# Token-mixer kernel: rows of the middle stage on every fourth partition, its tables in eight parts, stores ahead of loads

## Time and profile before

| | before |
|---|---|
| median of three runs | 3273.02 us |
| the profiled execution's own time | 3274.27 us |
| its span, first to last instruction | 3272.1 us |
| mean granted TensorE clock | 0.962 |
| TensorE busy | 2991.4 us (91%) |
| VectorE, GpSimd, ScalarE busy | 2595.4, 1578.9, 1297.7 us |
| first matmul of the middle stage | 384.57 us |
| first and last issue of a large store (L442) | 394.66 and 487.82 us |

### The profile page before, as it was taken

How to read it: one execution, slowest core, us unless ns; L and a number is a source line. 1 busy time by engine, 2 the same in 40 slices (tenths; PEclk the granted TensorE clock), 3 DMA queues, 4 the chain that set the end, 5 groups by cost and what they waited for, 6 DMA issues and landing times.

```text
span 3272.1 us, 58005 instructions
## 1 busy us (share of the span) xinstructions
PE 2991.4 (91%) x17218; PEld 2833.4 (87%) x17218; DVE 2595.4 (79%) x4304; ACT 1297.7 (40%) x2452; POOL 1578.9 (48%) x1527
## 2 busy tenths in 40 slices
PE   2555689999999799999999999999999999999999
PEld 2444438989898799999999999999999999999999
DVE  7999566777777888887878788787878788887776
ACT  1111235666667433333333333333333333333443
POOL 5666304666667544544545354444544454443221
PEclk7777799999999899999999999999999999999999
DMA  7656582332333466565656566565656565655443
GB/s 237 205 192 206 154 243 85 110 122 97 113 107 131 164 221 217 214 232 209 224 199 232 209 224 220 203 233 199 236 197 237 211 222 217 222 216 181 142 132 80
DMA packets 212157, 613.21 MB, mean 187 GB/s; under 512 B 19921, under 2 KB 61137, under 8 KB 210833
## 3 DMA queue, kind: packets, MB, share of 16 engines
q1 hardware_dynamic: 202304, 598.04, 52.6%
q10 hardware_dynamic: 9696, 13.37, 1.5%
HBM read 394.67 MB, written 216.66 MB: 187 GB/s over the span
## 4 chain that ended last, share of the span: by engine, by line
PE 75%; issue 8%; POOLq 6%; DVE 4%; DVEq 2%; DMA 2%; ACT 2%; POOL 1%; ACTq 0%; SPq 0%
PE banks L1570 55%; PE banks L1437 10%; POOLq L1042 5%; PE banks L1508 4%; PE banks L1510 2%; DVE zl L797 2%; PE banks L1494 2%; DMA m_scr<-mst 1%; DVEq L845 1%; POOL head L1040 1%; ACT zh L1261 1%; PE banks L1649 1%; DVE angle L785 0%; PE banks L1484 0%; DVE mst L749 0%
## 5 line engine op out<-in xcount | busy, mean ns | idle before, releaser
L1570 PE MATMUL banks<-zh,wh 128*128 128x384 f32 x3828 | 1295.1, 338 | 45.1 <-DVE rbuf L849 45.1
L1570 PE MATMUL banks<-zh,wl 128*128 128x384 f32 x3828 | 1282.1, 335 | 0.0
L1570 PE MATMUL banks<-zl,wh 128*128 128x384 f32 x3828 | 1281.3, 335 | 0.0
L849 DVE TENSOR_TENSOR rbuf<-rbuf,banks 128x384 f32<-128x384 f32 x1168 | 643.1, 551 | 253.5 <-PE banks L1570 216.4
L1570 PEld LDWEIGHTS banks<-zh,wh 128*128 128x128 f32 x3828 | 720.2, 188 | 67.2 <-DVE rbuf L849 47.5
L1570 PEld LDWEIGHTS banks<-zl,wh 128*128 128x128 f32 x3828 | 720.7, 188 | 0.0
L1570 PEld LDWEIGHTS banks<-zh,wl 128*128 128x128 f32 x3828 | 720.0, 188 | 0.0
L1074 POOL TENSOR_TENSOR wsum<-wraw 128x384 f32<-128x384 f32 x176 | 179.6, 1020 | 1107.6 <-DVE wl L792 982.2
L1253 ACT ACTIVATE wh<-wsum 128x384 fp32r<-128x384 f32 x704 | 370.2, 526 | 771.5 <-PE banks L1570 730.0
L792 DVE TENSOR_TENSOR wl<-wsum,wh 128x384 fp32r<-128x384 f32 x664 | 505.3, 761 | 39.1 <-ACT wh L1253 14.3
L1253 ACT ACTIVATE wh<-wraw 128x384 fp32r<-128x384 f32 x528 | 278.0, 527 | 498.5 <-PE banks L1570 498.5
(11 more groups left out here) (141 smaller groups left out, 4260.4 us busy)
## 6 DMA issues: line engine op xcount, KB each, us to landing
wraw<-w_pairs SPq DMA_DIRECT2D x176, 768.0 KB, 6.7
rbuf<-y_scr SPq DMA_DIRECT2D x176, 768.0 KB, 5.7
y_scr<-rbuf SPq DMA_DIRECT2D x160, 768.0 KB, 4.0
xin<-x_pad SPq DMA_DIRECT2D x22, 1728.0 KB, 9.5
z_scr<-zsc SPq DMA_DIRECT2D x33, 768.0 KB, 4.0
zraw<-z_scr SPq DMA_DIRECT2D x33, 768.0 KB, 7.4
x_scr<-x1s SPq DMA_DIRECT2D x22, 576.0 KB, 5.8
t_scr<-tst ACTq DMA_DIRECT2D x44, 288.0 KB, 4.1
```

Of the source, the lines that this page charges most:

```text
L849: dve.tensor_tensor(part, part, dst(k, i), ALU.add).then_inc(r_done, 1)
L1570: last = pe.matmul(dst, l[w][:, q, :], r[par][:, operand, q, :], start=starts and q == 0 and t == 0, stop=q == 2 and t == 2, skip_group_ch ...
```

## The change

- Rows: real row n (below 32) sits on partition 4 n, imaginary row n on 4 n + 1, and the two rows n = 32 on 2 and 3, in `traw`, in the tables (both sides) and in `mst`. `traw`, `mst` and the matmuls' operands and results are 128 partitions wide.
- Tables: `fall` is 128 partitions x 64 x 256 (8 MB) where it was 96 x 64 x 132 (3.1 MB). It is no longer loaded ahead of the first stage's loop: SP's loop is written out and loads an eighth (1 MB) at the end of each of its rounds 2 to 9.
- Memory: `mst1` takes the place of the raw weights `w1_raw`, `w2_raw` and `wt_raw`; ScalarE waits for `cwl_ready` before the middle stage.
- Stores: the large store becomes two DMAs of 384 KB, one for each of the real and imaginary results.
- Order: `load_t(g + 4)` is issued behind `store_b(g)`, and its own wait on `g_ready` is gone.
- VectorE's clearing (L740) covers all 128 partitions of `traw`.

```diff
+    place = np.array([4 * n + w if n < NT - 1 else 2 + w for w in range(2) for n in range(NT)])
+    f_rows = np.zeros((P, P // 2, 2, P))
...
-        traw = [alloc(T, f"traw{s}", [NRZ, 4, B, D]) for s in range(4)]
+        traw = [alloc(T, f"traw{s}", [P, 4, B, D]) for s in range(4)]
...
-        fall = alloc(C, "fall", [NRZ, P // 2, 2 * NR])
-        mst = [alloc(C, f"mst{s}", [NR, 4, B, D]) for s in range(2)]
-        w1_raw = alloc(C, "w1_raw", [P, 2, F])
+        fall = alloc(C, "fall", [P, P // 2, 2 * P])
+        mst = [alloc(C, "mst0", [P, 4, B, D])]
+        R = ExitStack()
+        w1_raw = alloc(R, "w1_raw", [P, 2, F])
+        w2_raw = alloc(R, "w2_raw", [P, HB, D])
+        wt_raw = alloc(R, "wt_raw", [P, 2, D])
+        R.close()
+
+        mst += [alloc(C, "mst1", [P, 4, B, D])]
...
             def load_t(g):
                 s = g % 4
                 for w in range(2):
-                    sp.dma_start(traw[s][64 * w:64 * w + 32].rearrange("p i b d -> p i (b d)"),
+                    sp.dma_start(traw[s][w:P:4].rearrange("p i b d -> p i (b d)"),
                                  t_scr[w, 0:NT - 1, 4 * g:4 * g + 4, :]).then_inc(b_in[s], 16)
-                sp.dma_start(traw[s][32:34].rearrange("p i b d -> p i (b d)"),
+                sp.dma_start(traw[s][2:4].rearrange("p i b d -> p i (b d)"),
...
+                tiles = m_scr[2 * g:2 * g + 2].rearrange("t (i w a) x -> w a (t i) x", i=2, w=2)
...
-                sp.dma_start(m_scr[2 * g:2 * g + 2].rearrange("t (i q) x -> q (t i) x", i=2), rows[0:64]).then_inc(out_b, 16)
-                sp.dma_start(m_scr[NT - 1:NT, 4 * g:4 * g + 4, :], rows[64:65]).then_inc(out_b, 16)
+                for w in range(2):
+                    sp.dma_start(tiles[w], rows[w:P:4]).then_inc(out_b, 16)
+                sp.dma_start(m_scr[NT - 1:NT, 4 * g:4 * g + 4, :], rows[2:3]).then_inc(out_b, 16)
...
-            sp.dma_start(fall[:], f_low).then_inc(f_in, 16)
...
-            with sp.Fori(1, NG) as g:
+            for g in range(1, NG):
                 for h in range(2):
                     load_a(g, h)
                     store_x1(g - 1, h)
+
+                if 1 < g < 10:
+                    part = slice(8 * (g - 2), 8 * (g - 1))
+                    sp.dma_start(fall[:, part], f_low[:, part]).then_inc(f_in, 16)
...
             for g in range(NGB):
-                if g + 4 < NGB:
-                    sp.wait_ge(g_ready, 4 * g + 4)
-                    load_t(g + 4)
...
                 store_b(g)
+                if g + 4 < NGB:
+                    load_t(g + 4)
...
-                dve.memset(traw[s][32:64], 0.0).then_inc(b_zero, 1)
+                dve.memset(traw[s][:], 0.0).then_inc(b_zero, 1)
...
+            act.wait_ge(cwl_ready, 5)
             step_b(0)
...
-            pe.wait_ge(f_in, 16)
+            pe.wait_ge(f_in, 128)
...
-                    pe.matmul(bank[2 * i][0:NR, 0:4 * (L + 2)], fall[:, q, 0:NR], traw[g % 4][:, i, :, 0:L + 2],
+                    pe.matmul(bank[2 * i][:, 0:4 * (L + 2)], fall[:, q, 0:P], traw[g % 4][:, i, :, 0:L + 2],
                               start=True, stop=True)
-                    pe.matmul(bank[2 * i + 1][0:NR, 0:4 * L], fall[:, q, NR:2 * NR], traw[g % 4][:, i, :, L:D],
+                    pe.matmul(bank[2 * i + 1][:, 0:4 * L], fall[:, q, P:2 * P], traw[g % 4][:, i, :, L:D],
```

More of the change, by code:

```diff
@@ L48 @@
 NPAIR = NT // 2
-NRZ = 96
-NR = 2 * NT
 NGB = P // 8
@@ L96, in fourier_constants @@
             f_low[1, :, i, 1, 1] = -np.sin(p2)
[L98 to L102, removed]
+    place = np.array([4 * n + w if n < NT - 1 else 2 + w for w in range(2) for n in range(NT)])
+    f_rows = np.zeros((P, P // 2, 2, P))
+    f_rows[place[:, None, None, None], np.arange(P // 2)[None, :, None, None], np.arange(2)[None, None, :, None],
+           place[None, None, None, :]] = f_low.reshape(2 * NT, P // 2, 2, 2 * NT)
     none = np.zeros((D2, D))
@@ L106, in fourier_constants @@
     return (f_seq.astype(np.float32), f_chan.astype(np.float32), f_rest.astype(np.float32),
-            f_rows.reshape(NRZ, P // 2, 4 * NT).astype(np.float32))
+            f_rows.reshape(P, P // 2, 2 * P).astype(np.float32))
 def row_order():
@@ L227, in token_fourier_mixer @@
         newton = alloc(C, "newton", [P, B])
-        fall = alloc(C, "fall", [NRZ, P // 2, 2 * NR])
-        mst = [alloc(C, f"mst{s}", [NR, 4, B, D]) for s in range(2)]
-        w1_raw = alloc(C, "w1_raw", [P, 2, F])
+        fall = alloc(C, "fall", [P, P // 2, 2 * P])
[6 more added lines that the diff above has]
+        mst += [alloc(C, "mst1", [P, 4, B, D])]
         w1t = alloc(C, "w1t", [P, F], F32R)
         wtt = alloc(C, "wtt", [P, D], F32R)
-        w2_raw = alloc(C, "w2_raw", [P, HB, D])
-        wt_raw = alloc(C, "wt_raw", [P, 2, D])
         C.close()
@@ L311, in stored @@
         def stored(k, groups):
-            return 48 * groups + (0 if k else 16)
+            return 64 * groups + (0 if k else 16)
         up_bank = (2, 3, 4, 5, 2, 3)
@@ L439, in store_b @@
                 rows = mst[g % 2][:].rearrange("p i b d -> p i (b d)")
+                tiles = m_scr[2 * g:2 * g + 2].rearrange("t (i w a) x -> w a (t i) x", i=2, w=2)
                 out_b = m_out[g % 2]
                 sp.wait_ge(m_ready, 4 * g + 4)
-                sp.dma_start(m_scr[2 * g:2 * g + 2].rearrange("t (i q) x -> q (t i) x", i=2), rows[0:64]).then_inc(out_b, 16)
-                sp.dma_start(m_scr[NT - 1:NT, 4 * g:4 * g + 4, :], rows[64:65]).then_inc(out_b, 16)
+                for w in range(2):
+                    sp.dma_start(tiles[w], rows[w:P:4]).then_inc(out_b, 16)
+                sp.dma_start(m_scr[NT - 1:NT, 4 * g:4 * g + 4, :], rows[2:3]).then_inc(out_b, 16)
                 if g == 0:
-                    sp.dma_start(m_scr[NT - 1:NT, P // 2:P // 2 + 1, :], rows[65:66, 0:1]).then_inc(out_b, 16)
-                    sp.dma_start(m_scr[NT - 1:NT, P - 3:P, :], rows[65:66, 3:0:-1]).then_inc(out_b, 16)
-                else:
-                    sp.dma_start(m_scr[NT - 1:NT, P - 3 - 4 * g:P + 1 - 4 * g, :], rows[65:66, ::-1]).then_inc(out_b, 16)
-            sp.dma_start(fall[:], f_low).then_inc(f_in, 16)
+                    sp.dma_start(m_scr[NT - 1:NT, P // 2:P // 2 + 1, :], rows[3:4, 0:1]).then_inc(out_b, 16)
+                    sp.dma_start(m_scr[NT - 1:NT, P - 3:P, :], rows[3:4, 3:0:-1]).then_inc(out_b, 16)
+                else:
+                    sp.dma_start(m_scr[NT - 1:NT, P - 3 - 4 * g:P + 1 - 4 * g, :], rows[3:4, ::-1]).then_inc(out_b, 16)
             sp.dma_start(w1_raw[:, 0, :], w1[0:P, :]).then_inc(cw_in, 16)
@@ L746, in group_b @@
                     even = mst[s % 2][:, i, :, 1:L]
-                    hpart = bank[2 * i + 1][0:NR, 0:4 * L].rearrange("p (b l) -> p b l", b=B)[:, :, 1:L]
+                    hpart = bank[2 * i + 1][:, 0:4 * L].rearrange("p (b l) -> p b l", b=B)[:, :, 1:L]
                     dve.tensor_tensor(mst[s % 2][:, i, :, D - 1:L:-1], even, hpart, ALU.subtract)
@@ L1200, in group_b @@
                     act.activation(mst[s % 2][:, i, :, 0:L + 1],
-                                   bank[2 * i][0:NR, 0:4 * (L + 2)].rearrange("p (b l) -> p b l", b=B)[:, :, 0:L + 1],
+                                   bank[2 * i][:, 0:4 * (L + 2)].rearrange("p (b l) -> p b l", b=B)[:, :, 0:L + 1],
                                    ACT.Copy).then_inc(g_evac, 1)
```

## The result

The changed kernel takes 3247.5 us (median of 4 runs, 3247.42 to 3249.16) against 3273.03 for the kernel before. The ratio is 0.9923, with a 95% interval of 0.9906 to 0.994. The profiled execution has a span of 3245.6 us, 26.5 less than before, and a mean granted TensorE clock of 0.968.

A forecast was written before the change was run, and what follows sets the result against it. VectorE was taken to pace the first stage, store landings the middle one, with TensorE busy 91% of the span. Terms -8.6, three zeros, -6.1 and +0.4 summed to -14.3 us, giving 3258.8 us; 8-in-10 range 3248 to 3267.

The forecast's parts named there:

- Step 1: First stage: without the table ahead of the loop, VectorE's wait for `win` goes, 24.06 to 15.43 us a half: -8.6 us.
- The rival in which this gain stays out: Start: SP may stick at the weights' many small packets as behind the table; 3267.4 us or part gain, chance 0.10.
- Steps 2 and 3: First stage, table in eight parts; middle stage, wider tiles: 0 each, both with bounds 0 and +5 us.
- Step 4: Middle stage's start: ScalarE's first copy waits for GpSimd's last splitting instruction, 0.3 us later, costing 0.
- Step 5: Middle stage: rows on every fourth partition and store before load, 6.21 to 5.80 us a group: -6.0 us.
- the sum: Total of -14.3 us; its +0.4 is the last store's second issue, delaying `load_u(2)` and the third stage.
- nothing comes of the middle stage: Middle stage: store stands behind the previous round's load, 6.21 us a group stays; 3264.8 us, chance 0.25.
- the spread doubles the rate: Middle stage: spread rows quicken transfers, TensorE binds at 5.33 us a group; -21.4 us in all, 3251.6 us, chance 0.27.

The follow-up runs named there:

- table-only kernel: Kernel before, with its 96-partition table loaded in eight parts at the end of rounds 2 to 9 instead of ahead of the loop: 3263.38 us.
- four blocks: Kernel before, table padded to 128 partitions and loaded ahead of the loop by four DMAs of 32 neighbouring partitions each: 3279.29 us.
- four strided DMAs: Kernel before, table padded to 128 partitions and loaded ahead of the loop by four DMAs, each on every fourth partition: 3268.04 us.

## Why the prediction was wrong, by its steps

**Step 1, the table leaves the start: right.** Forecast -8.6 us; `x1s` to `x1s` 24.06 to 15.09, and VectorE's last L714 of the stage, L719 now, moves from 354.82 to 346.18 us, 8.64 earlier. The table-only kernel gained 9.5 us by the medians (3272.85 for before on the same chip). The rival in which this gain stays out falls.

**Steps 2 and 3, eight parts and wider tiles: right.** No wait of VectorE for `win` after the start. In the middle stage all matmuls together average 509 and 497 ns with 128 x 128 weights against 522 and 507, probably because fewer of them run at the lower clock.

**Step 4, ScalarE's new wait: right in the cost, at a larger size.** ScalarE's first copy does start when GpSimd is done, at 377.72 us. The 8.1 us of its wait are counted from its own last instruction; before, it stood 7.87 us there for TensorE. What the new wait adds is the distance from the first matmul to the first copy, 4.28 us instead of 2.86: 1.4 us where I had 0.3, since the first operands come sooner, as the step had said. It costs nothing measurable: first matmul to first store is 10.08 us against 10.09.

**Step 5: the step that failed, twice.** Its words were "So spreading alone isn't shown to buy rate, and I keep 286 GB/s". And: "Ahead of the load it should take that", meaning the lone store's 6.34 us. I gave -6.1 us to the order (the step's heading has -6.0) and nothing to the spread. Measured, the order gives 0 and the spread 0.73 us a group, 10.7 to 11 us over the loop, with 1.1 us at the first load and 1.7 at the last store besides, where the sum had +0.4. The second error had its warning in the text. The rival "nothing comes of the middle stage" says that the store stands behind the load of the round before. For the order by itself it was the right one.

The first error is one of reading. I had 413 and 364 GB/s for transfers over all partitions, 223 for 32, and 216 for 96, and took the 96 as a point on the way from 32 to 128. It was a single row, and I had not asked what else could make it slow; it decided 0.33 against 0.27 between my forecast and the rival "the spread doubles the rate". That rival's 3251.6 us was 4 us too high. The floor is 5.21 us a group, not 5.33, since I had divided a busy time by the count of its records. The rival's sum also lacked the first load's landing, the last store's 1.7 us, the 1.34 us of the clock at the end of the first stage, and the 2.9 us behind the middle stage. The last two make some 4 of the profiled execution's 26.5 us that belong to no step: had they stayed out, the time would have fallen inside my range, with the mechanism just as wrong. On the other side, the loop didn't quite reach that floor: 5.50 on the average, with 82.43 - 15 x 5.21 = 4.3 us lost, all of it from the first `load_u` at 434.83 us on.

The window rates of 409 and 210 GB/s for the same bytes in the same number of DMAs show that placement decides the rate. By the Trainium skill (SBUF — State Buffer, section "Door 1: The DMA port swizzle"), partitions 0 to 63 share 8 ports and 64 to 127 the other 8. The four blocks, the four strided DMAs and the fall to 7.32 us with all rows in the lower half agree with that. The 96-partition table doesn't: two thirds of its partitions lie on the first 8 ports, so an estimate from the page's 218 GB/s for 8 ports is 218 x 3/2 = 327 GB/s, and the trace has 216. There the measurement decides, and the page's rule doesn't say all. Why 96 partitions move so slowly stays open.

## What to carry to other kernels

When a DMA moves fewer than 128 partitions, look at the GB/s of a stretch in which it runs alone, and not at the DMA share, which is near 1 at half the rate. Place the rows so that each DMA spreads evenly over all 128 partitions (96 neighbouring ones were no better than 32), and do it for loads and stores alike: one side alone brought at most half of the loop's gain here. Before the order of a queue is changed to shorten a landing, ask whether the DMA engines are full: with a share of 0.95 here, what went first only took the place of something else. When two traces differ by 1 us ahead of the stage that was edited, compare their granted clocks before the gain is given to a step. Last, a single row that speaks against a mechanism should be tested for its own cause before it outweighs two that speak for it.

## What was unexpected of the hardware

- 96 partitions at 33792 bytes each moved at 216 GB/s, 128 at 409. Padding a tile with a third more bytes made its load shorter.
- The gains of spread loads (0.1 us a group, within the variation) and of spread stores (0.4) don't add up to that of both (0.73); the cause stays open.
- Rows on 0 to 63 with operands and results alike gave 6.62 us a group, more than the old rows' 6.21, whose operands lay on 0 to 31 and 64 to 95, at the same DMA sizes.
